# Attention weights left unnormalised: the reciprocal row sums multiply the outputs instead

## The chip, the cores and the metric

One core of one Trainium2 chip runs the whole kernel. The metric is the time of one execution on the device in microseconds (us), the median of several. Engines: TensorE (PE; its weight loads are PEld), VectorE (DVE), ScalarE (ACT), GpSimd (POOL) and SyncE (SP), each with an instruction queue of its own in program order, tied to the others by semaphores (`wait_ge`, `then_inc`).

## The reference

Three layers, one behind the other, on 2 x 768 tokens: attention with 8 heads of 64 per batch, then a gated mixture of 8 experts, then a gated pair of products. Cut to what matters here:

```python
def _attn_ref(q, k, v, n_sink, window):            # q, k, v: (2, 8, 768, 64)
    scores = scale * np.matmul(q, k.transpose(0, 1, 3, 2))
    keep = is_sink | in_window                     # first 4 keys, and the last 128
    scores = np.where(keep, scores, -1000000000.0)
    a = np.exp(scores - np.max(scores, axis=-1, keepdims=True))
    a = a / (np.sum(a, axis=-1, keepdims=True) + 1e-09)
    return np.matmul(a, v)
...
x = attn_out.transpose(0, 2, 1, 3).reshape(B * S, H * D)
x = _moe_ref(x, w_gate, w1, w2)                    # sum over experts of P * (relu(x @ w1) @ w2)
return _moe2_ref(x, w_a, w_b, w_out)               # (x @ w_a) * (x @ w_b) @ w_out
```

## The kernel before

**Pairs of heads.** Attention is done for 8 pairs of heads, `p` = 0 to 7 (`PAIRS`), pair `p` being heads 2i and 2i+1 (`a` = 0, 1) of batch b, with `i, b = divmod(p, 2)`. A pair has 6 tiles of 128 queries (`j`, `QT`); a tile sees 128 keys (j = 0) or 272 (the tile before, 16 sink keys, its own). Scores of tile j stand in PSUM banks 2*(j%2)+a, so banks 0 to 3; turned probabilities in banks 4 and 5 (`T_BANK`); outputs of the two halves of the sequence in banks 6 and 7 (`O_BANK`), head a in partitions 64a to 64a+63. `pr` is a ring of 4 (two pairs of two heads) with probabilities, `esum` holds their row sums, queries in the partitions.

**One pair's way.** ScalarE and VectorE split q and k into a rounded high part (`split_pair_hi`, L956 and L958) and a low part (`split_pair_lo`, L1258 and L1261). PE multiplies them (`scores`, L541), VectorE scales, masks and takes minima (`mask_scores`, L1272), ScalarE takes the exponentials in place with their row sums (`exps`, L967). VectorE adds 1e-9 and takes reciprocals, for two tiles at a time (`row_sums` L1284, `reciprocals` L1289). POOL multiplies the probabilities of tiles 0 to 2 (0 and 1 for the last pair) by them (`normalise`, L424), VectorE those of tiles 3 to 5 (L1298). PE turns the probabilities by transposes in four steps (`turn`, L567); ScalarE copies head 0's, VectorE head 1's into `pt` (`copy_turned`, L976 and L1307). PE multiplies them by the values (`weigh`, L588; sink keys L595), the two halves one after the other. ScalarE copies the outputs out of PSUM into their rounded high part (L982, L985) and issues the DMAs for the values of pair p+2 from its own queue (L988, L989). VectorE takes low parts and differences from the outputs in PSUM (`output_step`, L1317 to L1331), ScalarE rounds the differences (`token_parts_hi`, L997 to L1000), POOL takes their low parts (`token_parts_lo`, L449 to L456). These differences are operands of the expert products, which are done with seven block products instead of eight (P1 to P7), each of three matmuls per k (high by high, low by high, high by low; L623 to L625).

**The order by hand.** Every engine runs `pair(p)` for p from -2 or -1 on, and in it works on three pairs at once: outputs of p, turning of p+1, scores, masks and exponentials of p+2, the split of p+3. On PE: `weigh(p)`, then four times a turning step of p+1 followed by the scores of two tiles of p+2. On ScalarE: outputs of p; four times a turn copy and the exponentials of two tiles; the split of p+3; the rounding of differences of p. On VectorE: four times a turn copy, an output step, the masks of two tiles with sums and reciprocals between; the split of p+3; the last reciprocals; the six multiplications of tiles 3 to 5 of p+2. POOL: multiplications of p, the sink columns of k for p+2 (L414), low parts of p-2.

**What follows.** Behind the last pair PE does the first half of the router's logits (`logits_of(0)`, 20 matmuls, L648) and begins the experts (`group(0, 0)`): P1, P5, P2, P6, P3, P7 for the first half of the hidden columns, P1 of the second half, P4. P6 waits until ScalarE has copied P1's result out of PSUM (`keep`, L1071). The weights are split too: POOL makes sums of weight blocks (`weight_sums(n, sub)`, L436 to L441), ScalarE rounds them (`ws_hi`, L948), VectorE takes the low parts (`ws_lo`, L1336). The order of POOL at the end of attention is `weight_sums(0, 0)`, low parts of pair 6, `weight_sums(0, 1)`, low parts of pair 7.

Of the kernel before, what the change touches and what calls it, by code (L numbers as in the profile page):

```python
# [25 lines left out]
P = 128  # L26
# [7 lines left out]
def build(nc, qT, kT, v, sizes, w_gate, w1, w2, w_a, w_b, w_out, out):  # L34
# [43 lines left out]
    with ctx:  # L78
# [36 lines left out]
        with ExitStack() as att:  # L115
# [7 lines left out]
            mask = sa("mask", [P, MW], F32)  # L123
            wgs = sa("wgs", [P, KC, P], F32R)
# [22 lines left out]
        with ExitStack() as router:  # L147
# [10 lines left out]
            "sink_zero", "normed", "normed_dve", "turned", "turn_act", "turn_dve", "pv_done", "out_hi", "out_lo",  # L158
# [34 lines left out]
        def pool_tiles(p):  # L193
            return QT - 4 if p >= PAIRS - 1 else QT - 3

        def pool_before(p):
            return sum(2 * pool_tiles(x) for x in range(p))
# [6 lines left out]
        S_BANK, T_BANK, O_BANK = 0, 4, 6  # L204
        L_BANK = ((4, 5), (6, 7))
# [183 lines left out]
        def _(pool):  # L389
# [28 lines left out]
            def normalise(p, tiles):  # L418
                for j in tiles:
                    pool.wait_ge(s["recip"], 3 * p + 1 + j // 2)  # L420
                    for a in range(2):
                        r = 2 * (p % B) + a
                        t = pr[:, r, start_of[j]:start_of[j] + width[j]]
# [18 lines left out]

            def token_parts_lo(p):

                i, b = divmod(p, B)
                k = i % 2
                if i < 2:
                    pool.wait_ge(s["t_hi"], p + 1)
                    nc.gpsimd.tensor_tensor(xol[:, 4, k, b, :], x32[:, 5, k, b, :],  # L449
                                            xoh[:, 4, k, b, :].bitcast(F32), ALU.subtract).then_inc(s["t_lo"], 1)  # L450
                else:
                    pool.wait_ge(s["t_hi"], 4 + 2 * (p - 4) + 1)
                    nc.gpsimd.tensor_tensor(xol[:, 5:7, k, b, :], x32[:, 5:7, k, b, :],
                                            xoh[:, 5:7, k, b, :].bitcast(F32), ALU.subtract)
                    pool.wait_ge(s["t_hi"], 4 + 2 * (p - 4) + 2)
                    ins = nc.gpsimd.tensor_tensor(xol[:, 2, k, b, :], x32[:, 2, k, b, :],  # L456
                                                  xoh[:, 2, k, b, :].bitcast(F32), ALU.subtract)
                    if i == KC - 1:
                        ins.then_inc(s["x_ready"], 1)
# [27 lines left out]
            with pool.If(fits == 1):  # L487
                for p in range(B):
# [35 lines left out]
        def _(pe):  # L524
            pe.wait_ge(s["const_ready"], 15)

            def scores(p, tiles):
# [3 lines left out]
                for j in tiles:  # L531
                    bank = S_BANK + 2 * (j % 2)
                    pe.wait_ge(s["masked"], 2 * QT * p + 2 * j + 2)
                    at = max(j - 1, 0) * PITCH
# [11 lines left out]
            def turn(p, q):  # L546
                i = TURN_ORDER[q]
                for a in range(2):
# [13 lines left out]
                    for j, src, dst in parts:  # L562
                        if j < pool_tiles(p):
                            pe.wait_ge(s["normed"], pool_before(p) + 2 * j + a + 1)
                        else:
                            pe.wait_ge(s["normed_dve"], p + 1)
                        mm = nc.tensor.transpose(ps[:, bank, dst:dst + P], pr[:, r, src:src + P], ident[:])  # L567
                    mm.then_inc(s["turned"], 1)

            def weigh(p):  # L570
# [3 lines left out]
                for bank in range(2):  # L574
                    if p > 0:
                        pe.wait_ge(s["out_lo"], p)
# [61 lines left out]
            def logits_of(pi):  # L638

                if pi == 0:  # L640
                    pe.wait_ge(s["x_ready"], 1)
                    pe.wait_ge(s["gate_lo"], 1)
# [65 lines left out]
            with pe.If(fits == 1):  # L708
# [12 lines left out]
                for p in range(-1, PAIRS - 1):  # L721
                    if p >= 0:
                        weigh(p)
                    pair(p)
                weigh(PAIRS - 1)

# [196 lines left out]
        def _(act):  # L923
# [54 lines left out]
            def outputs(p):  # L978
                i, b = divmod(p, B)
                k = i % 2  # L980
                act.wait_ge(s["pv_done"], 2 * p + 1)
                nc.scalar.copy(xoh[:, i // 2, k, b, :], ps[:, O_BANK, 0:HT]).then_inc(s["out_hi"], 1)  # L982
                act.wait_ge(s["pv_done"], 2 * p + 2)
# [816 lines left out]
```

## Time and profile before

| | |
|---|---|
| time, median of 3 runs | 1452.02 us (1451.71 to 1453.65) |
| the profiled execution: its own time | 1450.18 us |
| the profiled execution: span from first to last instruction | 1448.4 us |
| busy over the span | PE 1398.6 us (97%), DVE 808.4 (56%), ACT 501.5 (35%), POOL 223.7 (15%) |
| mean granted TensorE clock | 0.997 |

A timeline row reads: start in us from the beginning of the span, duration in us (of all that are merged in it), engine, line of the kernel, operation, output<-inputs, forms, how many; in brackets the idle time of the engine just before and what ended it. L12 is line 12 of the kernel. A windows row reads: stretch, its length, then busy us and number of instructions for PE, PEld, DVE, ACT and POOL, the granted TensorE clock as a share of 2.4 GHz, the share of DMA time, and GB/s. Row groups by line read: busy us in all and mean ns of one, then idle time before them and who ended it. Matmuls overlap, so one's duration is longer than the distance to the next.

### The profile page before, as it was taken

To read this page: it belongs to the slowest core of one execution; us is meant where nothing else is said; L and a number is where in the kernel's file an instruction comes from. 1 tells how busy PE (TensorE), PEld (TensorE's weight loads), DVE (VectorE), ACT (ScalarE), POOL (GpSimd) and SP (SyncE) were. 2 spreads that over 40 slices of the span, in tenths; PEclk is the share of its full clock that TensorE was granted. 3 is DMA by queue.
4 is the path that set the end of the run, shared out by engine and by line. 5 is a ranking of instruction groups with operands and counts; after the bars stand their busy time and mean duration, and the time that the engine had idled before them with its cause. 6 is when DMAs were issued, how large, how long until landed. Compare 5 with 4: busy or idle time off the path is not lost.

```text
span 1448.4 us, 20715 instructions
## 1 busy us (share of the span) xinstructions
PE 1398.6 (97%) x7400; PEld 1246.1 (86%) x7400; DVE 808.4 (56%) x1585; ACT 501.5 (35%) x1085; POOL 223.7 (15%) x289
## 2 busy tenths in 40 slices
PE   4877999999999999999999999999999999999999
PEld 3655889988889998889998888998888989999998
DVE  6898765645444453544545444454544666656665
ACT  5785232423223242222323222242322443232331
POOL 3355110101101010110101011010111321101100
PEclk9999999999999999999999999999999999999999
DMA  4311100001010000101001010000100001001002
GB/s 141 100 45 56 44 30 29 30 29 59 15 44 29 29 29 29 58 21 37 29 29 32 26 58 29 29 29 29 58 15 29 15 30 44 30 30 44 30 1 88
DMA packets 49724, 56.45 MB, mean 39 GB/s; under 512 B 2432, under 2 KB 37376, under 8 KB 49664
## 3 DMA queue, kind: packets, MB, share of 16 engines
q1 hardware_dynamic: 44768, 53.26, 11.3%
q10 hardware_dynamic: 4896, 2.41, 0.6%
q8 instruction: 36, 0.59, 0.2%
q14 instruction: 24, 0.20, 0.0%
HBM read 52.51 MB, written 3.15 MB: 38 GB/s over the span
## 4 chain that ended last, share of the span: by engine, by line
PE 86%; DVE 7%; ACT 4%; issue 2%; DMA 0%; DVEq 0%; ACTq 0%
PE ps L623 28%; PE ps L625 28%; PE ps L624 28%; ACT pr L967 2%; DVE pr L1298 1%; DVE st L1675 1%; DVE pr L1272 1%; DVE wsl L1336 1%; PE ps L693 1%; DVE pt L1307 1%; ACT pt L976 1%; PE ps L567 0%; ACT st L1139 0%; ACT hh L1146 0%; DVE acc L1714 0%
## 5 line engine op out<-in xcount | busy, mean ns | idle before, releaser
L623 PE MATMUL ps<-xoh,wsh 128*128 128x384 f32 x1232 | 414.9, 337 | 3.0 <-DVE xol L1579 2.1
L625 PE MATMUL ps<-xol,wsh 128*128 128x384 f32 x1232 | 412.7, 335 | 0.0
L624 PE MATMUL ps<-xoh,wsl 128*128 128x384 f32 x1232 | 412.3, 335 | 0.0
L623 PE MATMUL ps<-w2h,hh 128*128 128x512 f32 x912 | 360.7, 396 | 0.8 <-DVE acc L1557 0.8
L625 PE MATMUL ps<-w2l,hh 128*128 128x512 f32 x912 | 359.8, 395 | 0.0
L624 PE MATMUL ps<-w2h,hl 128*128 128x512 f32 x912 | 359.6, 394 | 0.0
L1562 DVE SCALAR_TENSOR_TENSOR acc<-ps,g_now,acc 128x512 f32<-128x512 f32 x180 | 135.1, 751 | 201.7 <-PE ps L625 201.7
L623 PEld LDWEIGHTS ps<-xoh,wsh 128*128 128x128 f32 x1232 | 231.3, 188 | 10.5 <-DVE st L1675 3.9
L624 PEld LDWEIGHTS ps<-xoh,wsl 128*128 128x128 f32 x1232 | 231.3, 188 | 3.7
L625 PEld LDWEIGHTS ps<-xol,wsh 128*128 128x128 f32 x1232 | 231.2, 188 | 0.0
L625 PEld LDWEIGHTS ps<-w2l,hh 128*128 128x128 f32 x912 | 171.7, 188 | 39.8
L623 PEld LDWEIGHTS ps<-w2h,hh 128*128 128x128 f32 x912 | 171.9, 188 | 37.0 <-DVE acc L1557 1.2
L624 PEld LDWEIGHTS ps<-w2h,hl 128*128 128x128 f32 x912 | 171.8, 188 | 35.7
L436 POOL TENSOR_TENSOR sst<-raw 128x256 f32<-128x256 f32 x44 | 32.5, 738 | 1037.6 <-DVE wsl L1336 1037.6
L1071 ACT COPY st<-ps 128x384 f32<-128x384 f32 x96 | 46.0, 480 | 373.7 <-PE ps L625 373.7
L1535 DVE TENSOR_TENSOR st<-ps,st 128x384 f32<-128x384 f32 x96 | 53.4, 557 | 122.2 <-PE ps L625 122.2
L1535 DVE TENSOR_TENSOR ab<-ps,ab 128x384 f32<-128x384 f32 x96 | 53.5, 558 | 85.0 <-PE ps L625 84.9
L1543 DVE SCALAR_TENSOR_TENSOR hl<-ps,hh 128x384 fp32r<-128x384 f32 x64 | 35.7, 557 | 77.2 <-ACT hh L1084 76.7
L1336 DVE TENSOR_TENSOR wsl<-raw,wsh 128x512 fp32r<-128x512 f32 x88 | 63.8, 739 | 17.4 <-ACT wsh L948 17.4
L948 ACT CAST wsh<-raw 128x512 fp32r<-128x512 f32 x88 | 52.0, 621 | 55.2 <-POOL raw L438 55.2
L1084 ACT ACTIVATE hh<-ps 128x384 fp32r<-128x384 f32 x64 | 31.5, 491 | 106.1 <-PE ps L625 106.1
L1071 ACT COPY ab<-ps 128x384 f32<-128x384 f32 x96 | 46.1, 480 | 55.6 <-PE ps L625 55.6
(142 smaller groups left out, 1337.8 us busy)
## 6 DMA issues: line engine op xcount, KB each, us to landing
raw<-in_w_dram SPq DMA_DIRECT2D x32, 512.0 KB, 3.4
raw<-in_w_dram SPq DMA_DIRECT2D x16, 1024.0 KB, 5.1
rk<-in_k_dram SPq DMA_DIRECT2D x8, 384.0 KB, 4.0
rq<-in_q_dram SPq DMA_DIRECT2D x8, 384.0 KB, 4.9
raw<-in_w_a_dram SPq DMA_DIRECT2D x6, 512.0 KB, 3.6
raw<-in_w_b_dram SPq DMA_DIRECT2D x6, 512.0 KB, 3.6
raw<-in_w_out_dram SPq DMA_DIRECT2D x6, 512.0 KB, 3.5
out_dram<-acc SPq DMA_DIRECT2D x12, 256.0 KB, 2.0
```

The source lines that it names most:

```text
L436: nc.gpsimd.tensor_tensor(s1, a21, a22, ALU.add).then_inc(s["s_sum"], 1)
L623: nc.tensor.matmul(o, ah, bh, start=first, stop=False, skip_group_check=True)
L624: nc.tensor.matmul(o, al, bh, start=False, stop=False, skip_group_check=True)
L625: return nc.tensor.matmul(o, ah, bl, start=False, stop=last, skip_group_check=True)
L948: nc.scalar.copy(ws_piece(wsh, sub, j), ws_raw(sub, j)).then_inc(s["w_hi"], 1)
L967: nc.scalar.activation(t, t, ACT.Exp, bias=nmin[:, r, j:j + 1], scale=-1.0, accum_out=esum[:, r, j:j + 1]).then_inc(s["exped"], 1)
L1071: nc.scalar.copy((st, ab)[sub][:, slot, :], ps[:, bank_of(sub, name), 0:HT]).then_inc(s["kept"], 1)
L1084: nc.scalar.activation(hh[:, 2 * sub + 1, 0, :], ps[:, bank_of(sub, "P4"), 0:HT], ACT.Relu)\
L1336: nc.vector.tensor_tensor(ws_piece(wsl, sub, j), ws_raw(sub, j), ws_piece(wsh, sub, j).bitcast(F32), ALU.subtract)\
L1535: nc.vector.tensor_tensor(t, ps[:, bank_of(sub, name), 0:HT], t, ALU.add).then_inc(s["c_add"], 1)
L1543: nc.vector.scalar_tensor_tensor(out=hl[:, 2 * sub + m, half, :], in0=src, scalar=0.0, in1=hh[:, 2 * sub + m, half, :].bitcast(F32), op0=A ...
L1562: ins = nc.vector.scalar_tensor_tensor(out=acc[:, tile, :], in0=ps[:, Y_BANK + k % 2, :], scalar=g_now[:, tile:tile + 1], in1=acc[:, tile, ...
```

## The change

Nothing divides the probabilities any more: PE turns the exponentials as they are (`turn` waits for `exped`). Sums and reciprocals are done once for a pair, for all six tiles, `esum` then holding the reciprocals. A new step on PE, `widen(p)`, ahead of `weigh(p)`, has 12 matmuls whose weight is a column of `esum` broadcast to 64 columns and whose moved operand is the identity: the result has in the 64 rows of a head the reciprocal of each query's sum along the columns, in banks 2 and 3, which the scores of odd tiles use too (they wait for `wide_in`). VectorE begins `pair(p)` with `scale_outputs(p)`: it copies the 128x768 reciprocals into a new buffer `wide`, then multiplies the two halves of the outputs by it, from PSUM into `x32`. ScalarE rounds these from `x32` (one copy before its first turn copy, for p from 4 on another behind it), and issues the value DMAs behind the first turn copy. The differences of outputs and their low parts go from VectorE to POOL for p up to 5 (`output_sums`, `outputs_lo`), and stay on VectorE for the last two pairs (`output_sum`), where VectorE also takes the low parts of pair 6's differences; POOL takes the low parts of the outputs of pairs 6 and 7 behind `weight_sums(0, 0)` and ahead of `weight_sums(0, 1)`. POOL copies the sink columns three pairs ahead instead of two. The general path for other sizes is not run with these inputs.

```diff
@@ POOL
-            def normalise(p, tiles):
-                for j in tiles:
-                    pool.wait_ge(s["recip"], 3 * p + 1 + j // 2)
-                    for a in range(2):
...
-                        nc.gpsimd.tensor_scalar(t, t, esum[:, r, j:j + 1], None, ALU.mult)\
-                            .then_inc(s["normed"], 1)
+            def outputs_lo(p):
+                i, b = divmod(p, B)
+                k = i % 2
+                pool.wait_ge(s["out_hi"], p + 1)
+                pool.wait_ge(s["t_sum"], t_sums_before(p + 1))
+                ins = nc.gpsimd.tensor_tensor(xol[:, i // 2, k, b, :], x32[:, i // 2, k, b, :],
+                                              xoh[:, i // 2, k, b, :].bitcast(F32), ALU.subtract)
+                if i >= 2:
+                    ins = nc.gpsimd.tensor_tensor(xol[:, 3, k, b, :], x32[:, 3, k, b, :],
+                                                  xoh[:, 3, k, b, :].bitcast(F32), ALU.subtract)
+                ins.then_inc(s["out_lo"], 1)
+
+            def output_sums(p):
...
+                pool.wait_ge(s["scaled"], 2 * p + 2)
+                if i < 2:
+                    nc.gpsimd.tensor_tensor(t12, b12, early, ALU.subtract).then_inc(s["t_sum"], 1)
+                else:
+                    nc.gpsimd.tensor_tensor(t12, b22, t12, ALU.subtract).then_inc(s["t_sum"], 1)
+                    pool.wait_ge(s["t_sum"], t_sums_before(p) + 1)
+                    nc.gpsimd.tensor_tensor(t4, early, t12, ALU.subtract).then_inc(s["t_sum"], 1)
+                    nc.gpsimd.tensor_tensor(b12, b22, b12, ALU.subtract).then_inc(s["t_sum"], 1)
...
-                for p in range(PAIRS):
-                    own = range(pool_tiles(p))
-                    normalise(p, own[:2])
-                    if p + 2 < PAIRS:
-                        sink_columns(p + 2)
-                    normalise(p, own[2:])
-                    if p >= 2:
-                        token_parts_lo(p - 2)
+                for p in range(PAIRS - 2):
+                    if p + 3 < PAIRS:
+                        sink_columns(p + 3)
+                    output_sums(p)
+                    outputs_lo(p)
+                    token_parts_lo(p)
                 pool.wait_ge(s["qk_lo"], 2 * PAIRS)
                 weight_sums(0, 0)
-                token_parts_lo(PAIRS - 2)
+                outputs_lo(PAIRS - 2)
+                outputs_lo(PAIRS - 1)

             weight_sums(0, 1)
             token_parts_lo(PAIRS - 1)
@@ PE
-                        if j < pool_tiles(p):
-                            pe.wait_ge(s["normed"], pool_before(p) + 2 * j + a + 1)
-                        else:
-                            pe.wait_ge(s["normed_dve"], p + 1)
+                        pe.wait_ge(s["exped"], 2 * QT * p + 2 * j + a + 1)
...
+            def widen(p):
+                pe.wait_ge(s["recip"], p + 1)
+                pe.wait_ge(s["masked"], 4 + 2 * QT * min(p + 2, PAIRS))
+                for j in range(QT):
+                    at = j % 3 * P
+                    for a in range(2):
+                        r = 2 * (p % B) + a
+                        rows = slice(D * a, D * a + D)
+                        mm = nc.tensor.matmul(ps[rows, WIDE_BANK + j // 3, at:at + P],
+                                              esum[:, r, j:j + 1].to_broadcast([P, D]), ident[:],
+                                              start=True, stop=True, skip_group_check=True)
+                mm.then_inc(s["recip_wide"], 1)
@@ ScalarE
+                    if p >= 0 and q == 0:
+                        outputs_hi(p, True)
+                        next_values(p)
@@ VectorE
-            def normalise(p):
-                dve.wait_ge(s["recip"], 3 * p + 3)
-                for j in range(pool_tiles(p), QT):
-                    for a in range(2):
...
-                        ins = nc.vector.tensor_scalar(t, t, esum[:, r, j:j + 1], None, ALU.mult)
-                ins.then_inc(s["normed_dve"], 1)
+            def scale_outputs(p):
+                i, b = divmod(p, B)
+                k = i % 2
+                dve.wait_ge(s["recip_wide"], p + 1)
+                nc.vector.tensor_copy(wide[:], ps[:, WIDE_BANK:WIDE_BANK + 2, 0:HT]).then_inc(s["wide_in"], 1)
+                dve.wait_ge(s["wide_in"], p + 1)
+                for half, place in enumerate((i // 2, 2 + i // 2)):
+                    dve.wait_ge(s["pv_done"], 2 * p + half + 1)
+                    nc.vector.tensor_tensor(x32[:, place, k, b, :], ps[:, O_BANK + half, 0:HT], wide[:, half, :],
+                                            ALU.mult).then_inc(s["scaled"], 1)
...
             def pair(p):
+                if p >= 0:
+                    scale_outputs(p)
                 for q in range(4):
                     if p >= 0 and p + 1 < PAIRS:
                         copy_turned(p + 1, q)
-                    if p >= 0:
-                        output_step(p, q)
+                    if p >= PAIRS - 2:
+                        output_sum(p, q)
...
                 if p + 2 < PAIRS:
-                    row_sums(p + 2, 2)
+                    row_sums(p + 2)
                 if 2 <= p + 3 < PAIRS:
                     split_pair_lo(p + 3)
                 if p + 2 < PAIRS:
-                    reciprocals(p + 2, 2)
-                    normalise(p + 2)
+                    reciprocals(p + 2)
+                if p == PAIRS - 2:
+                    token_parts_lo(p)
```

## Rows read from the trace of the kernel before

**Rows 1.** The page: its first line and the chain that ended last, by engine.
```profile
span 1448.4 us, 20715 instructions
...
PE 86%; DVE 7%; ACT 4%; issue 2%; DMA 0%; DVEq 0%; ACTq 0%
```

**Rows 2.** Windows of all engines, then of PE alone: busy us, clock, DMA.
```profile
0.00:133.00 133.00, 93.18 (x780) 68.28 (x780) 110.71 (x376) 88.81 (x267) 58.14 (x88) 0.97 0.29 89
...
59.00:60.00 1.00, 1.00 (x7) 0.50 0.00 0
...
104.00:105.00 1.00, 0.00 (x0) 1.00 0.00 0
...
107.00:108.00 1.00, 1.00 (x13) 0.50 0.00 0
```

**Rows 3.** Timeline of ScalarE: start, duration, what it ran, idle time before it.
```profile
41.88 0.40 ACT L967 ACTIVATE pr<-pr,nmin 128x128 f32<-128x128 f32 x1 [0.82 <-DVE nmin L1272]
...
70.22 0.40 ACT L967 ACTIVATE pr<-pr,nmin 128x128 f32<-128x128 f32 x1 [1.90 <-DVE nmin L1272]
...
79.88 0.38 ACTq L988 DMA_DIRECT2D vs<-in_v_dram  x1
...
80.95 0.59 ACT L976 COPY pt<-ps 128x512 f32<-128x512 f32 x1 [0.59 <-PE ps L567]
...
83.99 0.40 ACT L967 ACTIVATE pr<-pr,nmin 128x128 f32<-128x128 f32 x1 [2.46 <-DVE nmin L1272]
...
113.24 0.40 ACT L967 ACTIVATE pr<-pr,nmin 128x128 f32<-128x128 f32 x1 [0.87 <-DVE nmin L1272]
...
144.11 0.84 ACT L1071 COPY st<-ps 128x384 f32<-128x384 f32 x2
```

**Rows 4.** Timeline of VectorE.
```profile
24.11 2.53 DVE L1298 TENSOR_SCALAR pr<-pr,esum 128x272 f32<-128x272 f32 x6
...
78.34 1.02 DVE L1258 TENSOR_TENSOR w2l<-rq,w2h 128x768 fp32r<-128x768 f32 x1 [0.71 <-ACT w2h L956]
...
80.44 2.25 DVE L1298 TENSOR_SCALAR pr<-pr,esum 128x272 f32<-128x272 f32 x6
...
82.60 0.68 DVE L1307 COPY pt<-ps 128x512 f32<-128x512 f32 x1
...
83.20 0.54 DVE L1317 TENSOR_TENSOR xol<-ps,xoh 128x384 fp32r<-128x384 f32 x1
...
121.23 6.04 DVE L1298 TENSOR_SCALAR pr<-pr,esum 128x272 f32<-128x272 f32 x8
```

**Rows 5.** Groups by line and form, 0 to 150 us.
```profile
L1307 DVE COPY pt<-ps 128x512 f32<-128x512 f32 x24 | 16.4, 683 | 2.7 <-PE ps L567 2.7
...
L456 POOL TENSOR_TENSOR xol<-x,xoh 128x384 fp32r<-128x384 f32 x4 | 5.0, 1255 | 0.0
...
L1307 DVE COPY pt<-ps 128x384 f32<-128x384 f32 x8 | 4.4, 545 | 2.2 <-PE ps L567 1.9
```

**Rows 6.** Timeline of PE.
```profile
36.94 0.39 PE L595 MATMUL ps<-pt,vz 128*64 128x128 f32 x4
37.16 1.47 PE L588 MATMUL ps<-pt,vs 128*64 128x128 f32 x16
...
58.05 1.82 PE L567 MATMUL ps<-ident,pr 128*128 128x128 f32 x8 [0.82 <-ACT pt L976]
...
93.53 1.09 PE L567 MATMUL ps<-ident,pr 128*128 128x128 f32 x8
...
138.06 0.45 PE L648 MATMUL ps<-xoh,wgs 128*128 128x384 f32 x1 [0.66 <-POOL xol L456]
...
149.20 0.44 PE L623 MATMUL ps<-xoh,wsh 128*128 128x384 f32 x1
```

**Rows 7.** Timeline of POOL.
```profile
121.86 1.96 POOL L453 TENSOR_TENSOR xol<-x,xoh 128x768 fp32r<-128x768 f32 x1 [1.89 <-ACT xoh L999]
...
138.96 0.74 POOL L436 TENSOR_TENSOR sst<-raw 128x256 f32<-128x256 f32 x1 [0.96 <-DVE wsl L1336]
```

More of the change, by code:

```diff
@@ L123, in build @@
             mask = sa("mask", [P, MW], F32)
+            wide = sa("wide", [P, 2, HT], F32)
             wgs = sa("wgs", [P, KC, P], F32R)
@@ L191, in build, with t_sums_before, t_parts_before @@
         TURN_ORDER = (0, 1, 3, 2)
[L193 to L197, printed above, removed]
+        def t_sums_before(p):
+            return min(p, 2 * B) + 3 * max(p - 2 * B, 0)
+        def t_parts_before(p):
+            return min(p, 2 * B) + 2 * max(p - 2 * B, 0)
         def chosen(eng):
@@ L204, in build @@
         S_BANK, T_BANK, O_BANK = 0, 4, 6
+        WIDE_BANK = 2
         L_BANK = ((4, 5), (6, 7))
@@ L441, in weight_sums @@
                 nc.gpsimd.tensor_tensor(s4, a12, s2, ALU.subtract).then_inc(s["s_sum"], 1)
+            def outputs_lo(p):
[12 more added lines that the diff above has]
+                k = i % 2
+                early, b12, b22, t12, t4 = (x32[:, o, k, b, :] for o in (i // 2, 2, 3, 5, 6))
+                pool.wait_ge(s["scaled"], 2 * p + 2)
[6 more added lines that the diff above has]
+                    nc.gpsimd.tensor_tensor(b12, b22, b12, ALU.subtract).then_inc(s["t_sum"], 1)
             def token_parts_lo(p):
@@ L533, in scores @@
                     pe.wait_ge(s["masked"], 2 * QT * p + 2 * j + 2)
+                    if j == 1 and p >= 2:
+                        pe.wait_ge(s["wide_in"], p - 1)
                     at = max(j - 1, 0) * PITCH
@@ L722, in _ @@
                     if p >= 0:
+                        widen(p)
                         weigh(p)
                     pair(p)
+                widen(PAIRS - 1)
                 weigh(PAIRS - 1)
+                pe.wait_ge(s["wide_in"], PAIRS)
             def unit_product(name, n, sub, pi):
@@ L976, in copy_turned, with outputs_hi, next_values @@
                 nc.scalar.copy(pt[:, 0, i, 0:w], ps[:, T_BANK, 0:w]).then_inc(s["turn_act"], 1)
-            def outputs(p):
+            def outputs_hi(p, late):
                 i, b = divmod(p, B)
                 k = i % 2
-                act.wait_ge(s["pv_done"], 2 * p + 1)
-                nc.scalar.copy(xoh[:, i // 2, k, b, :], ps[:, O_BANK, 0:HT]).then_inc(s["out_hi"], 1)
-                act.wait_ge(s["pv_done"], 2 * p + 2)
-                late = x32[:, 2, k, b, :] if i < 2 else xoh[:, 3, k, b, :]
-                nc.scalar.copy(late, ps[:, O_BANK + 1, 0:HT]).then_inc(s["out_hi"], 1)
+                if not late:
+                    act.wait_ge(s["scaled"], 2 * p + 1)
+                    ins = nc.scalar.copy(xoh[:, i // 2, k, b, :], x32[:, i // 2, k, b, :])
+                    if i < 2:
+                        ins.then_inc(s["out_hi"], 1)
+                elif i >= 2:
+                    act.wait_ge(s["scaled"], 2 * p + 2)
+                    nc.scalar.copy(xoh[:, 3, k, b, :], x32[:, 3, k, b, :]).then_inc(s["out_hi"], 1)
+            def next_values(p):
+                i, b = divmod(p, B)
                 if i + 1 < KC:
+                    act.wait_ge(s["pv_done"], 2 * p + 2)
                     cols = slice((i + 1) * P, (i + 2) * P)
@@ L1003, in pair @@
                 if p >= 0:
-                    outputs(p)
+                    outputs_hi(p, False)
                 for q in range(4):
@@ new lines, in output_sum @@
+            def output_sum(p, x):
+                i, b = divmod(p, B)
+                k = i % 2
+                early, b12, b22, t12, t4 = (x32[:, o, k, b, :] for o in (1, 2, 3, 5, 6))
+                if x == 0:
+                    dve.wait_ge(s["scaled"], 2 * p + 2)
+                    dve.wait_ge(s["t_lo"], p - 3)
+                    nc.vector.tensor_tensor(t12, b22, t12, ALU.subtract).then_inc(s["t_sum"], 1)
+                elif x == 1:
+                    dve.wait_ge(s["t_sum"], t_sums_before(p) + 1)
+                    nc.vector.tensor_tensor(t4, early, t12, ALU.subtract).then_inc(s["t_sum"], 1)
+                elif x == 2:
+                    nc.vector.tensor_tensor(b12, b22, b12, ALU.subtract).then_inc(s["t_sum"], 1)
```

73 lines of the change are left out of this document (27 added, 46 removed).

## The prediction, made before the change was run

> **What bounds the kernel now.** I read the page first: the chain of work that ended last is TensorE for 86% of a span of 1448.4 us, VectorE for 7%, ScalarE for 4%, and names no POOL [rows 1]. Then the windows: from 0 to 133 us, where attention is, PE is busy 93.18 of 133 us, VectorE 110.71, ScalarE 88.81 [rows 2]. So the diff can only act on when the stream of expert products begins; behind it everything moves by the same amount. Then the timelines of the three engines, to find the loop that sets a round (one head pair). I mark a round by the first exponential on ScalarE: 41.88, two rounds on 70.22, then 83.99 and, two rounds on, 113.24 us [rows 3]. A plain round is 13.77 us (70.22 to 83.99). It alternates: exponentials and turn copies on ScalarE until the q split of a later pair lets VectorE start its low part 8.12 us after the mark (78.34 against 70.22); the two low parts and the reciprocals take it to 80.40 [rows 3, 4]; six multiplications of probabilities on VectorE take 2.25 us (from 80.44), and the turn copy (0.60 from start to next start), one output subtraction (0.47) and the first masked scores (0.3) lead to the next mark [rows 4, 5]. POOL's multiplications and PE lie beside this. PE's first 8 transposes begin 9.54 us after a mark (93.53) and take about 1.03, while VectorE asks for them 12.38 after it (82.60): a slack of 1.8 us [rows 4, 6].
>
> **The steady round after.** Removed from this loop: the 2.25 us of multiplications and the 0.47 us output subtraction. Added on VectorE behind the reciprocals (10.2 us after the mark): a copy of 128x768 from PSUM. Copies of 128x512 and 128x384 take 683 and 545 ns [rows 5]; 138 ns for 128 elements makes about 0.95 us; bounds 0.68 (as for 512) and 1.09 (two of 384). It must land before the product reads it, then a product of 0.54 us [rows 4] gives the first half at 11.75. The second product costs 0.47, the turn copy 0.60, the first mask 0.3: VectorE would reach the mark at 13.1. ScalarE now waits for the first product instead of for PE: its copy 0.45 us (11.8 to 12.25), then the turn copy, and behind it the two value DMAs, moved from before the turn copy to after it. Those two issues hold ScalarE 1.05 us from the start of the instruction they are issued under (79.88 to 80.95) [rows 3]. This gives 13.3: ScalarE decides by 0.2 us. From the fifth pair on there is a second rounding copy there, 0.45 us: 13.75. If the issue is hidden a round is 13.1.
>
> PE gains 12 spreading matmuls a round, 64 columns wide, 128 moved. The trace has no such instruction with a broadcast weight; the nearest are the sink products of 128x128, 4 records (2 matmuls, one for each head) in 0.22 us from 36.94 to 37.16 [rows 6]. Twelve are six such pairs, 1.3 us. The first transposes then end near 11.7 us after the mark instead of 10.6, and VectorE asks for them at 12.2 (behind both products): 0.5 us of slack is left. If the two halves did not run together it is about 3.0 us, by 24 records at 0.13 us, the spacing of the 8 transposes of 128 [rows 6]. Nothing below 1.3 is likely; I take 1.3. The small sum and reciprocal instructions go from six to two, and lie under ScalarE's exponentials: nothing. The POOL work removed (46 multiplications) isn't in the chain [rows 1]: nothing. The POOL work added (one to three differences, low parts) lies after the products; its consumer, ScalarE's rounding of differences, comes 9 us later: nothing, except where it meets VectorE at the end.
>
> **The sum, stage by stage.** Start: the multiplications for pair 0 hold VectorE 2.53 us from 24.11 [rows 4]; without them the masks of pair 1 start 2.5 us earlier. Then the first spreading matmuls stand ahead of the first weighing and here PE has no slack, so 0.6 comes back. First mark 40.0, that is -1.9. Three plain rounds: before 42.11 (the first two 28.34, 0.8 over two plain ones: they hold a stretch where the granted clock was 0.50, the 1.2 GHz level [rows 2]), after 39.9: -2.2. Two late rounds: before 83.99 to 113.24, 29.25; after 27.5: -1.75. Mark at 107.4.
>
> The last pairs: before, the eight multiplications of the last pair took 6.04 us (against 2.25 for six), because POOL's subtractions from 121.86 on and VectorE's instructions with SBUF operands stood in each other's way, up to 127.27 [rows 4, 7]. After, the exponentials end at 114.4, ScalarE's roundings take 1.2 and the first weight piece 0.6; VectorE's weight piece then waits for POOL's 128x768 subtraction, about 117.5, and ends 118.2. Broad copy 0.95, products 1.0, turn copy 0.6: 120.7. Three more turn rounds of about 1.1, spreading 1.3 and weighing 3.3: 128.6. PE starts the first logits at 128.7 instead of 138.06 [rows 6]: -9.4.
>
> Not all of that stays. After the last weighing the order is: VectorE copy, two products, three differences, done near 132.6. POOL takes the low parts of the last outputs (two; 128x384 takes 1255 ns on average where VectorE meets it, I take 2.2 for both), and only then the sums of weights for the second half, four at 0.75 us [rows 5, 7]. Before, these sums stood ahead of the last token parts and began at 138.96, 0.9 us after the logits [rows 7]. With two waits of 0.6 us behind VectorE they now end near 139.1. ScalarE is in order: it rounds the last weight piece (0.8), and only then keeps P1 (0.45), which the fourth product P6 waits for. That is 140.35. PE reaches P6 after 20 logit matmuls (3.5 us) and three products (3.1 us): 135.3. It waits 5.05 us. Before, the keep began at 144.11 [rows 3] and P6 was reached at 138.06 + 6.6 = 144.7: no wait. So -9.4 becomes -4.4; the 0.3 us that PE then waited before the product at 149.20 [rows 6] is gone too: -4.7.
>
> **A pause of 5 us.** At 104 to 105 us PE did nothing, and at 107 to 108 its granted clock was 0.50, the 1.2 GHz level; at 59 to 60 it was low behind a wait of under 1 us [rows 2]. A longer pause makes a fall likelier. By the second such case, where 8 transposes took 1.82 us instead of 1.09 and two rounds 0.8 longer [rows 3, 6], a fall costs at least 0.8 us; I take twice that, 1.7, since PE alone would be the bound here. I take this in: -4.7 + 1.7 = -3.0 us.
>
> The Trainium skill (TensorE: Matmul & The Clock Gate, section "What's actually happening") says that TensorE's clock falls to 1.2 GHz when it has been idle long enough and comes back after sustained work. By it the fall is certain and the result -3.0; without the rule the sum would be -4.7. The trace is partly with it: the pause at 104 was followed by the low level, but the fall at 58 had no such pause ahead of it.
>
> The sum is made against the profiled execution (span 1448.4 us, its own time 1450.18 us). The median of the runs is 1452.02, so I forecast 1449.0 there, 1447.2 for a profiled execution like this one.
>
> **Rivals.** (a) The last stall is short: POOL and VectorE hardly meet, the clock stays, the issue of DMAs is hidden. Then 1.2 (POOL without its waits) and 1.7 (clock) come back, and five rounds at 13.1 instead of 13.3 give 1.0: -6.9 us, 1445.1. For it: VectorE's first product could start before POOL's work. Against: the weight sums stand behind the last outputs in POOL's order whatever the speeds. (b) The freed time is taken by the new order altogether: the opening stall is longer by 2 to 3 us, since each difference on VectorE and POOL waits for the other as in the 6.04 us row. Then -1 to 0 us, 1451.5: no measurable change. For it: that row. Against: it was three POOL instructions in a row. (c) Slower: the spreading matmuls aren't paired and become the bound. At 3.0 us the 1.7 more exceed the 0.5 of slack by 1.2, and the mark comes at 12.2 + 1.2 + 0.9 = 14.3 (turn copy and mask behind it), five of them +5.0, the start and the last weighing +1.7 each, of which the POOL chain carries all: -3.0 + 8.4 = +5.4 us, 1457.4. It decides from 1.8 us on (slack used up), and is slower than before from about 2.1. For it: a broadcast weight is unknown here. Against: pairs of head halves do overlap in the weighing rows. (d) That the probabilities' multiplications were hidden anyway is excluded by the chain: VectorE's six of them lie on it in each round.
>
> **Numbers.** My forecast 0.5 (own range 1447.0 to 1451.0); (a) 0.2; (b) 0.2; (c) 0.1. A measurement tells about 0.2%, 2.9 us. The forecast lies at that border; half of it and all of (a), and a little of the early gains, count as faster: 0.52; same: 0.35, from the rest of the forecast and (b); slower: 0.13, (c) and a longer stall than in (b). The range reaches from (a) to somewhat over no change: 1444.8 to 1453.2.
>
> **What would show it.** Rounds of 13.3 us between marks for plain pairs (14 or more: (c), 13.1: issue hidden); six pairs of spreading matmuls in 1.3 us; PE's first logit matmul near 128.7; a wait of PE of about 5 us at the fourth product, released by ScalarE's copy of P1, behind POOL's weight sums; a granted clock of 0.5 behind it; from then on the same span. The prediction is wrong if that wait is under 2 or over 8 us, if VectorE's copy of 768 takes over 1.3 us, or if a round is set by PE.

## The result, and the profile after

The changed kernel takes 1443.64 us, median of 4 runs (1443.19 to 1445.95), against 1451.87 us for the kernel before in 4 runs (1450.96 to 1453.65): a ratio of 0.995, 95% interval 0.9938 to 0.9962, or 8.2 us less. The forecast was 1449.0 us and its range ended at 1444.8, so the gain is larger than the range allowed. The profiled execution of the changed kernel took 1445.95 us, the longest of its four, and its span is 4.3 us shorter than in [rows 1]. One execution, of 2309.79 us at a mean granted clock of 0.562 (experiment 8, the others there 0.995 to 0.998), is left out of all medians and intervals.

The page: first line and the chain that ended last.
```profile
span 1444.1 us, 21020 instructions
...
PE 88%; DVE 5%; ACT 5%; issue 2%; POOL 0%; DMA 0%; DVEq 0%; POOLq 0%
```
Windows, of all engines and then of PE alone, for [rows 2].
```profile
0.00:133.00 133.00, 103.81 (x1042) 83.92 (x1043) 100.58 (x309) 91.29 (x272) 44.10 (x66) 1.00 0.30 93
...
137.00:142.00 5.00, 5.00 (x16) 0.50 0.33 108
```
In the first 133 us VectorE is busy for 10 us less, and PE for 10.6 us more, since the spreading matmuls, the first logits and the first expert products lie inside the stretch. The low clocks of [rows 2] at 59 and 107 us are gone: from 0 to 130 us the mean granted clock is 1.00 in all seven profiles of kernels with the change, and 0.97, 0.97 and 0.99 in the three without it (before, experiments 4 and 8). The 0.8 us that the low clock had added to the first two rounds before are part of the gain. A new stretch at half clock, the 1.2 GHz level, stands at 137 to 142.

Timeline of ScalarE, for [rows 3]: the marks, and the instructions ahead of one.
```profile
40.06 0.40 ACT L1004 ACTIVATE pr<-pr,nmin 128x128 f32<-128x128 f32 x1 [0.78 <-DVE nmin L1321]
...
64.35 0.51 ACT L1020 CAST xoh<-x 128x384 fp32r<-128x384 f32 x1 [2.30 <-DVE x L1353]
64.44 0.38 ACTq L1032 DMA_DIRECT2D vs<-in_v_dram  x1
64.77 0.58 ACT L1013 COPY pt<-ps 128x512 f32<-128x512 f32 x1
64.85 0.56 ACTq L1033 DMA_DIRECT2D vz<-in_v_dram  x1
65.62 0.40 ACT L1004 ACTIVATE pr<-pr,nmin 128x128 f32<-128x128 f32 x1 [0.27 <-DVE nmin L1321]
...
78.39 0.40 ACT L1004 ACTIVATE pr<-pr,nmin 128x128 f32<-128x128 f32 x1 [0.27 <-DVE nmin L1321]
...
103.79 0.56 ACTq L1033 DMA_DIRECT2D vz<-in_v_dram  x1
103.80 0.51 ACT L1025 CAST xoh<-x 128x384 fp32r<-128x384 f32 x1
104.40 0.40 ACT L1004 ACTIVATE pr<-pr,nmin 128x128 f32<-128x128 f32 x1
```
The marks are at 40.06, 52.84, 65.62, 78.39, 91.40 and 104.40. A plain round is now 12.78 us, 13.77 before. In it the DMA issues that were to hold ScalarE run in the shadow of its rounding and its turn copy, from 64.44 to 65.41; ScalarE then idles 0.27 us and is released by VectorE's mask. The two late rounds take 13.0. There the second rounding stands behind the turn copy, and the second issue ends at 104.35, 0.05 us ahead of the mark: ScalarE doesn't idle, and the mark comes 0.55 us after the start of VectorE's mask (103.85) instead of 0.32.

Timeline of VectorE in the same round, for [rows 4].
```profile
60.87 0.96 DVE L1307 TENSOR_TENSOR wsl<-rq,wsh 128x768 fp32r<-128x768 f32 x1 [0.92 <-ACT wsh L993]
61.74 1.03 DVE L1310 TENSOR_TENSOR wsl<-rk,wsh 128x848 fp32r<-128x848 f32 x1
62.70 0.22 DVE L1334 RECIPROCAL esum<-esum 128x12 f32<-128x12 f32 x1
62.83 0.89 DVE L1349 COPY wide<-ps 128x768 f32<-128x768 f32 x1
63.76 1.02 DVE L1353 TENSOR_TENSOR x<-ps,wide 128x384 f32<-128x384 f32 x2
64.70 0.68 DVE L1342 COPY pt<-ps 128x512 f32<-128x512 f32 x1
65.30 0.28 DVE L1321 CUSTOM_DVE_ANT_0 pr<-ps,mask 128x128 f32<-128x128 f32 x1
```
Only the first carries a wait in brackets, for ScalarE's rounding of q; from there to the mask at 65.30 VectorE works without a wait. So a plain round has two parts: ScalarE's, 8.0 us from the mark at 52.84 to the end of that rounding, without idle time and about as long as before (8.12), and VectorE's, 4.75 us from there to the next mark. In the rest of this text "VectorE decides" is meant of this second part.

Timeline of PE, for [rows 6]: the spreading matmuls, the first logits, the first wait among the expert products, and the logits turned, the last instruction that I use to measure what attention and opening cost together.
```profile
58.67 1.53 PE L598 MATMUL ps<-ident,esum 128*64 128x128 f32 x24
60.00 1.28 PE L621 MATMUL ps<-pt,vs 128*64 128x256 f32 x12
...
127.10 0.41 PE L682 MATMUL ps<-xoh,wgs 128*128 128x384 f32 x1 [1.15 <-DVE wide L1349]
...
133.62 0.34 PE L658 MATMUL ps<-xol,wsh 128*128 128x384 f32 x1
136.74 0.69 PE L656 MATMUL ps<-xoh,wsh 128*128 128x384 f32 x1 [2.78 <-ACT st L1120]
137.23 0.52 PE L657 MATMUL ps<-xoh,wsl 128*128 128x384 f32 x1
...
154.22 0.94 PE L690 MATMUL ps<-ident,lt 40*128 40x40 f32 x12 [0.52 <-DVE lt L1419]
```
The 24 records of twelve spreading matmuls take 1.33 us to the next group. The first logits come 10.96 us earlier than in [rows 6]. P6, the fourth product, waits 2.78 us, and behind the wait matmuls stand 0.32 us apart instead of 0.17.

What the wait was for is read from the chain between 128.9 and 136.7 us: start, duration, what.
```profile
128.93 0.48 DVE x L1369
...
130.51 1.01 POOL xol L447
131.52 1.16 POOL sst L431
...
134.25 1.20 POOL sst L436
...
135.48 0.83 ACT wsh L985
136.31 0.39 ACT st L1120
```
This is the chain that the prediction described: VectorE's last difference, POOL's low parts, POOL's sums of weights, ScalarE's rounding of the last weight piece, and only then its copy of P1.

Where the time went, by stages (forecast, and measured, against the profiled execution of before):

| place | before | after | forecast shift | measured shift |
|---|---|---|---|---|
| first mark | 41.88 | 40.06 | -1.9 | -1.8 |
| mark of the last pair | 113.24 | 104.40 | -5.85 | -8.8 |
| first logit matmul | 138.06 | 127.10 | -9.4 | -11.0 |
| P6 begins | 144.76 | 136.74 | -4.4 | -8.0 |
| logits turned | 159.71 | 154.22 | -3.0, with the clock's fall | -5.5, with it |

The last 1.2 us between -5.5 and the span's -4.3 lie far behind the change, where this execution has a stretch at a lower granted clock (mean 0.91 from 1165 to 1185 us). The low clock behind P6's wait costs this execution 2.8 us, nearly all of it in 18 matmuls at 0.32 us instead of 0.17. Without it the shift would be -8.3 us.

### The profile page after: what moved, and what is told of

Its sections match the earlier page's. It is cut to its first block, busy times and chain, and to the rows that moved or that the text cites. A ratio compares the mean times of both kernels' runs of the same rounds, so it can differ in the third digit from the quotient of the medians.

```text
span 1444.1 us, 21020 instructions
## 1 busy us (share of the span) xinstructions
PE 1404.1 (97%) x7592; PEld 1258.3 (87%) x7592; DVE 789.1 (55%) x1507; ACT 499.1 (35%) x1081; POOL 206.0 (14%) x263
## 4 chain that ended last, share of the span: by engine, by line
PE 88%; DVE 5%; ACT 5%; issue 2%; POOL 0%; DMA 0%; DVEq 0%; POOLq 0%
PE ps L656 29%; PE ps L658 28%; PE ps L657 28%; ACT pr L1004 2%; DVE st L1722 1%; ACT pt L1013 1%; PE ps L727 1%; DVE wide L1349 0%; PE ps L586 0%; ACT st L1188 0%; DVE pr L1321 0%; ACT hh L1195 0%; DVE wsl L1385 0%; DVE acc L1761 0%; DVE x L1353 0%
```

## The experiments

The theory from these rows: three terms were off. Rounds are set by VectorE at 12.78 us, not by ScalarE at 13.3, so the stream begins 3 us earlier (experiments 5 and 6). P6's wait is set by POOL's order (2 and 3). The fall of the clock that the forecast took in happens in a part of the executions only (1, and the others beside it). Rivals: ScalarE does decide (then 6 shortens a round and 5 does nothing); the gain has little to do with the division (4); it comes from POOL and VectorE meeting less (8); PE's new work is near its limit (7). The first four ran beside a kernel before of 1451.33 us, the others beside 1451.25 us; the changed kernel itself was not measured again beside 5 to 8.

**1. The changed kernel again, five executions.** No edit.

> The changed kernel once more, unchanged. Theory A: the gain is the sum of the stages seen in its trace, 11.0 us by the first logit matmul, less a pause of 2.8 us ahead of the fourth product, 8.0 to 8.3 us in a run in which the clock stays at 2.4 GHz behind the pause. In the one trace so far it fell to 1.2 GHz and 18 matmuls went at 0.32 us instead of 0.173, 2.6 us. Then the times have two levels, about 1443.5 and 1446. Rival B: the fall is a constant part of the change, and the lower times come from elsewhere: one level, and every profile has the slow stretch.

1442.42 us (1440.78 to 1443.75), ratio 0.9936 (0.9923 to 0.995). The same pause at P6 (2.81 us), and in the profiled execution (1443.75 us) the same fall: 0.83 is the mean clock from 130 to 150 us. The five have two levels, 2.7 us apart, though lower than expected: 1443.75 and 1443.52 us with a mean granted clock of 0.998, 1440.78 and 1441.02 with 1.000, and 1442.42 between them with 0.999. A fall like the profiled one, 5.8 us at half clock, lowers the mean by 0.002. So one and the same kernel runs with the fall and without it. With 1.000 there was no full one; that the low clock of 1443.52 stands at P6 too isn't shown. The four executions of the first measurement have 0.996 (the profiled one, with its two stretches), 0.999, 0.997 and 0.998.

**2. The sums of weights ahead of the last outputs on POOL.**

```diff
@@ POOL
                 weight_sums(0, 0)
                 outputs_lo(PAIRS - 2)
+                weight_sums(0, 1)
                 outputs_lo(PAIRS - 1)
-            weight_sums(0, 1)
```

> POOL makes the sums of the second weight half before the low parts of the last pair's outputs instead of after them. Theory A: these sums, rounded by ScalarE ahead of its copy of P1, are what PE waits for at the fourth product. The pause of 2.8 us goes, and with it the fall of the clock: 1440.8 us, 2.8 under the changed kernel. Rival C: ScalarE's own queue (rounding the last pair's outputs and differences) holds the copy of P1: then the pause shrinks by at most 1 us, 1443. Rival D: VectorE's low parts of the weights become the next wait, at the first product of the second half: a pause of 1 to 2 us there, 1442.

1440.70 us (1439.35 to 1441.0), ratio 0.9926 (0.9913 to 0.994), 1.7 us under the changed kernel measured beside it and the fastest of those that divide. Timeline of PE in this kernel, from the first logits to the logits turned, all rows with a wait:
```profile
126.07 0.41 PE L683 MATMUL ps<-xoh,wgs 128*128 128x384 f32 x1 [1.15 <-DVE wide L1350]
...
138.10 0.44 PE L657 MATMUL ps<-xoh,wsh 128*128 128x384 f32 x1 [1.01 <-DVE st L1583]
...
148.62 0.94 PE L691 MATMUL ps<-ident,lt 40*128 40x40 f32 x12 [0.53 <-DVE lt L1420]
```
The wait for P1's copy is gone, and so is the low clock (mean 1.00 from 130 to 150). From the first logits to their turning it is 22.55 us, 27.12 in the changed kernel: 2.8 less wait, 2.7 less fall, 1.0 given back in a wait for VectorE's combinations that the first wait had covered. The order of two POOL calls is shown to be the cause of the pause. In the medians 1.7 us come of it and not 4.6: 2.8 less 1.0 is what is left where the changed kernel doesn't have the fall, and by the clocks in 1 at least two of its five executions have no full one.

**3. The same, and PE's wait for the wide copy behind the logits.**

```diff
@@ PE
                 weigh(PAIRS - 1)
-                pe.wait_ge(s["wide_in"], PAIRS)
...
             logits_of(0)
+            with pe.If(fits == 1):
+                pe.wait_ge(s["wide_in"], PAIRS)
             group(0, 0, opening=True)
```

> As the kernel with the weight sums first, and PE's wait for VectorE's broad copy of the last pair stands behind the first logit matmuls instead of ahead of them (they write other banks). Theory A: the first logit matmul starts 1.1 us earlier, and if nothing waits in the opening the whole 1.1 us stay: 1439.7 us. Rival C: ScalarE's copy of P1 is now the bound, and the 1.1 us come back as a wait at the fourth product: same as without this edit.

1440.86 us (1440.01 to 1440.9), ratio 0.9927 (0.9914 to 0.9941): nothing gained over 2. The logits begin at 125.30 with no wait, and the time is lost again at three places of PE's timeline:
```profile
132.55 0.44 PE L657 MATMUL ps<-xoh,wsh 128*128 128x384 f32 x1 [0.39 <-ACT st L1122]
136.20 0.44 PE L657 MATMUL ps<-xoh,wsh 128*128 128x384 f32 x1 [0.23 <-DVE wsl L1387]
138.57 0.44 PE L657 MATMUL ps<-xoh,wsh 128*128 128x384 f32 x1 [1.04 <-DVE st L1584]
```
So in this order the 1.15 us wait for the wide copy, which the prediction had overlooked, cost nothing by itself: behind it the other engines are late by as much. (The marks of this execution lie 0.45 us later than in 2, and so do the logits turned: 149.09 against 148.62.)

**4. The kernel before without any division.** The calls of `normalise` are left out of the kernel before, so the outputs are never divided by the row sums.

```diff
-                    normalise(p, own[:2])
...
-                    normalise(p, own[2:])
...
-                            pe.wait_ge(s["normed_dve"], p + 1)
+                        pe.wait_ge(s["exped"], 2 * QT * p + 2 * j + a + 1)
...
-                    normalise(p + 2)
```

> The kernel before, with the multiplications of the probabilities left out and nothing put in their place: the outputs are not divided by the row sums, which changes the results. It is the change's removal alone. Theory A: on VectorE a round loses 2.25 us, 13.77 to 11.5, or stops near 11.7 where ScalarE's own work sets it; the start gains 2.5, the last pair about 6. In all 2.5 + 5 x 2.2 + 5 = 18 us: 1434 us, so that what the change adds costs about 10 us. Rival: the multiplications were largely hidden or PE sets the round at once: less than 10 us faster than before.

1437.21 us (1434.68 to 1437.85), ratio 0.99 (0.9885 to 0.9915), 14.1 us less than before. Plain rounds are 12.07 us and the last one 13.69. This is the whole price that the division had on the path, to within 1 or 2 us: the four executions lie between 1434.68 (mean clock 1.000) and 1437.85 (0.998), and the profiled one has low clocks of its own (0.97 from 0 to 130 us). The change gets 8.2 to 8.9 of it and gives 5 to 6 back in the wide copy, the two products and the spreading; I had thought that it was 18 and 10.

**5. The value DMAs issued ahead of the first turn copy.**

```diff
@@ ScalarE
                     outputs_hi(p, False)
+                    next_values(p)
                 for q in range(4):
...
                         outputs_hi(p, True)
-                        next_values(p)
```

> The changed kernel with the two value DMAs issued where the kernel before issues them, ahead of ScalarE's first turn copy. The prediction's step: the issues hold ScalarE 1.05 us wherever they stand, so the round (ScalarE's chain decides) stays the same. Theory A: where the change puts them they run under the copies and cost nothing, VectorE decides the round (12.78 us) and ScalarE has 0.27 us to spare; ahead of the turn copy they push it and PE's second transposes back by about 0.5 us: round 13.0 and up to 1.2 us slower in all, 1444.8.

1444.37 us (1444.01 to 1447.51), ratio 0.996 (0.9945 to 0.9975). Timeline of ScalarE:
```profile
64.96 0.51 ACT L1020 CAST xoh<-x 128x384 fp32r<-128x384 f32 x1 [2.31 <-DVE x L1353]
64.96 0.38 ACTq L1032 DMA_DIRECT2D vs<-in_v_dram  x1
65.38 0.56 ACTq L1033 DMA_DIRECT2D vz<-in_v_dram  x1
66.03 0.59 ACT L1013 COPY pt<-ps 128x512 f32<-128x512 f32 x1 [0.56 <-issue]
66.52 0.40 ACT L1004 ACTIVATE pr<-pr,nmin 128x128 f32<-128x128 f32 x1
```
Now ScalarE does decide in plain rounds too: it idles 0.56 us in the issue, the exponential waits for nothing else, and marks are 13.07 to 13.18 us apart in plain rounds, 13.5 or 13.6 in late ones. From first to last mark it is 66.5 us against 64.3. What the forecast took for the changed order belongs to this one, and even here it is 13.1 and not 13.3. The time alone would not show it, since it lies among those of the changed kernel; the marks do.

**6. The first rounding of outputs behind the turn copy.**

```diff
@@ ScalarE
-                if p >= 0:
-                    outputs_hi(p, False)
                 for q in range(4):
...
                     if p >= 0 and q == 0:
+                        outputs_hi(p, False)
                         outputs_hi(p, True)
```

> The changed kernel with ScalarE's rounding copy of the first output half put behind its first turn copy instead of ahead of it. The prediction's step: ScalarE's chain (first product, rounding, turn copy, DMA issue) decides the round, so the turn copy starts 0.45 us earlier, but the sum of ScalarE's work ahead of the exponentials is unchanged. Theory A: VectorE decides (copy, two products, turn copy, mask), so a round stays at 12.78 us and the total at 1443.6, within 0.5. Rival: PE's second transposes, which wait for ScalarE's turn copy, decide something: 0.3 to 0.5 us a round faster, 1441.5.

1442.57 us (1441.93 to 1443.74), ratio 0.994 (0.9925 to 0.9955). In plain rounds ScalarE is done 0.3 us earlier, its idle time before the mark grows from 0.27 to 0.56, and the round stays at 12.78:
```profile
65.80 0.40 ACT L1004 ACTIVATE pr<-pr,nmin 128x128 f32<-128x128 f32 x1 [0.56 <-DVE nmin L1320]
...
78.57 0.40 ACT L1004 ACTIVATE pr<-pr,nmin 128x128 f32<-128x128 f32 x1 [0.56 <-DVE nmin L1320]
...
90.97 0.56 ACTq L1033 DMA_DIRECT2D vz<-in_v_dram  x1
91.57 0.40 ACT L1004 ACTIVATE pr<-pr,nmin 128x128 f32<-128x128 f32 x1 [0.37 <-DVE nmin L1320]
```
With 5 this settles who sets the plain round: VectorE, by about 0.3 us. The late rounds stay at 13.0, and the last two rows say why. The second rounding is over at 91.20 here, and VectorE's mask began at 91.02, which by the 0.33 us of plain rounds would allow a mark at 91.35. The mark comes at 91.57, 0.04 us after the end of the second issue, though the bracket names VectorE. So in late rounds the issues in ScalarE's queue do decide, by 0.2 us.

**7. The spreading matmuls done twice.**

```diff
@@ PE
-                for j in range(QT):
+                for j in tuple(range(QT)) * 2:
```

> The changed kernel with the 12 spreading matmuls of a pair done twice (same result). They take 1.33 us in the trace. PE's first transposes end 0.3 us before VectorE asks for them. Theory A: each round is longer by 1.33 - 0.3 = 1.0 us, six rounds with the first, and the last weighing by 1.3: about 7 us slower than the changed kernel, 1450.9. This is the size the third rival of the prediction (unpaired matmuls) would have had. Rival: PE is not near the bound, and less than 2 us are lost.

1449.90 us (1447.95 to 1451.58, ten runs), ratio 0.9991 (0.9982 to 1.0): 1.3 us under the kernel before, where the changed one is 8.2 to 8.9 under it. PE's timeline:
```profile
60.49 2.84 PE L598 MATMUL ps<-ident,esum 128*64 128x128 f32 x48
63.13 1.28 PE L621 MATMUL ps<-pt,vs 128*64 128x256 f32 x12
```
48 records take 2.64 us, so 24 cost 1.31. The plain round becomes 13.90, 1.12 longer: of the slack that PE had, 0.5 by the forecast, 0.2 was there. PE and VectorE are almost equally late in the changed kernel.

**8. The kernel before, with POOL's last subtractions held until VectorE's multiplications are done.**

```diff
@@ POOL (kernel before)
+                    if p == PAIRS - 1:
+                        pool.wait_ge(s["normed_dve"], PAIRS)
                     if p >= 2:
                         token_parts_lo(p - 2)
```

> The kernel before, with one wait added: POOL takes the low parts of pair 5 (and what follows) only when VectorE has multiplied the last pair's probabilities. Theory A: the 6.04 us of those eight multiplications are mostly waits for POOL; alone they take about 2.5, PE turns the last pair 3.5 us earlier, and POOL, 4 us later with its low parts and weight sums, gives part of it back at the first weight piece: 1 to 3 us faster than before, 1450. Rival: the multiplications are as slow without POOL: no gain, or 2 us slower because POOL's work is late.

1450.00 us (ten runs of 1447.29 to 1452.06), ratio 0.9991 (0.9982 to 1.0). VectorE's timeline, for the last of [rows 4]:
```profile
121.85 2.26 DVE L1300 TENSOR_SCALAR pr<-pr,esum 128x272 f32<-128x272 f32 x8
```
The eight multiplications take 2.26 us instead of 6.04, so POOL beside them was the cause of the 3.8 us. The first logits come at 136.07 instead of 138.06, with the last mark 0.6 later than in [rows 3]. The time falls by 1.3 us, which is just at the edge of the noise (0 to 2.6 by the interval). Perhaps that much of the change's gain was to be had without it.

**The clock behind the same pause.** Five profiled executions have PE's pause of 2.78 to 2.81 us at P6. Their granted clock and the time from P6 to the logits turned:

| kernel | mean clock, 130 to 150 us | from P6 to the logits turned |
|---|---|---|
| changed | 0.83 | 17.48 us |
| 1, changed again | 0.83 | 17.45 |
| 6, rounding behind | 0.91 | 16.27 |
| 5, DMAs ahead | 1.00 | 14.66 |
| 7, spreading twice | 1.00 | 14.66 |

The row of PE's windows of the changed kernel, and behind it that of 5.
```profile
130.00:150.00 20.00, 17.22 (x83) 0.83 0.08 27
```
```profile
130.00:150.00 20.00, 17.19 (x100) 1.00 0.14 46
```
PE is busy for the same 17.2 of 20 us and does 100 matmuls in it instead of 83. The fall costs 2.8 us where it is full, 1.6 where it is shorter (in 6, from about 137.9 to 141.2), and nothing where it doesn't come. These are four kernels, and in the two without a fall P6 also stands later (139.11 and 143.03 us, the others 136.05 to 136.74); that it isn't the kernel that decides is said by the mean clocks in 1, not by this table.

## Why the prediction was wrong, by its steps

The direction and the chain up to P6 were forecast; which engine sets a plain round, and the size, were not: -3.0 us forecast, -8.2 measured. The sum of the corrections is worked out at P6's beginning, since everything behind it moves with it.

- **Steady round: the step that failed.** "This gives 13.3: ScalarE decides by 0.2 us." VectorE decides, with 12.78. Two errors went into it. The two DMA issues were taken to hold ScalarE for 1.05 us from the start of the turn copy. They do take that long, but in plain rounds they begin under the rounding ahead of it (rounding from 64.35, issues from 64.44 to 65.41), so they are over 0.21 us before the mark and cost nothing; experiment 5 puts them ahead of the turn copy and pays 0.3 to 0.4 us a round. And VectorE's items were summed 0.3 us too long, to 13.1: the wide copy begins 9.99 us after the mark, not 10.2, and from its start at 62.83 to the mark it is 2.79 where 0.95 + 0.54 + 0.47 + 0.60 + 0.3 made 2.9. In late rounds ScalarE does decide, as forecast, but with 13.0 and not 13.75: the first product ends 0.3 us earlier than forecast, and the second rounding (0.45 in the sum) runs beside the issues and not behind them. Three plain rounds end 1.6 us earlier than forecast and two late ones 1.5, together 3.1 (64.34 us from first to last mark, 67.4 forecast), and so do the logits' inputs and POOL's chain: -3.0 us, the first mark having come 0.1 late. Rival (a) had a part of this in it, with 13.1 and 1.0 us.
- **The opening's wait: right in place, cause and order, wrong in size.** Forecast 5.05 us with P6 at 140.35; measured 2.78 with P6 at 136.74. P6 came 3.6 us earlier, 3.0 by the rounds and 0.6 because POOL's low parts took 2.0 (forecast 2.2), the sums 3.96 (3 and two waits, 4.2) and the rest of the chain a little less. PE was at P6 only 1.3 us earlier than forecast (133.96 against 135.3), because of the overlooked 1.15 us wait for the wide copy; so the wait shrank by 2.3. It is the position of P6, not the length of the wait, that enters the sum.
- **The clock: taken as certain, and it isn't.** 1.7 us were taken in. The fall came behind the pause as said and cost 2.8 us in the changed kernel (1.7 forecast), but two of five profiles with the same pause have none, and two of five executions of the changed kernel have a mean clock of 1.000. The term should have had a chance of its own. The Trainium skill (TensorE: Matmul & The Clock Gate, section "What's actually happening") says that the gate's own timing runs freely and isn't tied to the kernel. By that the same pause may or may not be followed by a fall, and the five profiles agree; its rule that idleness drops the clock was read in the prediction as if it were certain.
- **The sum.** For the logits turned in the profiled execution, which has the fall: -3.0 forecast, -3.0 for the rounds, -0.6 for the chain behind them, +1.1 for a fall of 2.8 and not 1.7, together -5.5 us; measured -5.5. Without a fall it would be -8.3. That the medians differ by nearly this, 8.2, is in part luck: by their clocks some of the four executions can have a fall, and the median before lies 1.7 us above the profiled execution from which the sum was made. How the 2.7 us between -5.5 and -8.2 are shared between the two isn't shown.
- **What held.** The start (-1.8 for -1.9). The spreading matmuls in pairs, 1.33 us for 1.3, so rival (c)'s premise is excluded; its threshold, slower from 2.1 us on, was too low with the rest of the sum: with 2.64 us in experiment 7 the kernel isn't slower than before. The wide copy, 0.91 us on average for 0.95. Nothing contradicts that POOL's multiplications and the small instructions cost nothing, but neither was tested by itself. That the division lay on the path: without any of it the time is 14.1 us less and a plain round 1.7 (experiment 4), which excludes (d).
- **The meeting of POOL and VectorE.** The forecast counted the 6.04 us as a loss that the change removes; experiment 8 shows that it was one, of which 2.0 us arrive at the first logits and about 1.3 in the time. It overlooked that the same meeting stands in the rounds. VectorE's timeline of before, in the last round:
```profile
108.14 3.80 DVE L1298 TENSOR_SCALAR pr<-pr,esum 128x272 f32<-128x272 f32 x6
```
Six multiplications take 3.80 us here, beside POOL's low part of 128x768 from 107.68 on, and 2.25 in plain rounds, also beside a POOL low part (79.60 to 81.17). At the pace of experiment 8, eight in 2.26, six would take 1.7, by estimate; so a part of the 2.25 in the prediction's loop is the meeting too. In the changed kernel they still meet, on VectorE's timeline here, but for less than (b) supposed:
```profile
113.35 1.48 DVE L1385 TENSOR_TENSOR wsl<-raw,wsh 128x512 fp32r<-128x512 f32 x1 [1.59 <-ACT wsh L985]
...
122.99 1.36 DVE L1379 TENSOR_TENSOR xol<-x,xoh 128x384 fp32r<-128x384 f32 x1
124.27 0.68 DVE L1385 TENSOR_TENSOR wsl<-raw,wsh 128x512 fp32r<-128x512 f32 x1
```
The weight piece takes 1.48 us beside POOL and 0.68 without it, and the subtraction of 128x384 takes 1.36 where others of that size take 0.56. The Trainium skill (SBUF — State Buffer, section "Who interferes with whom") names the port pair that VectorE and GpSimd share as the only place of contention. The 2.26 us of experiment 8 against 6.04 agree that the two hinder each other; that it is the only such place no run here shows.

Open is what decides whether the pause is followed by a fall, and how often it is: the mean clocks of nine executions are too few to count by. That the issues hold the late rounds is read from the rows of two kernels (the changed one and 6); a run with the issues taken out of late rounds alone was not made.

## What to carry to other kernels

When two engines finish a round within 0.3 us of each other by your sum, work out both cases as forecasts of their own, since an error in it is multiplied by the number of rounds; here the rounds were 3 of the 5.2 us that the forecast missed, about half in the plain ones. A DMA issue cost ScalarE's queue here only what no running instruction covered: look at what runs while it is issued and at what stands ahead of it, not at its own duration. The same two issues cost nothing in plain rounds, 0.2 us in late ones, with one more copy in the queue, and 0.3 to 0.4 ahead of the turn copy. When loop-end work moves between engines, write out the in-order queue of each engine at the join: the fastest version here differs from the change in the order of two calls on an engine that the chain hardly names.

## What the hardware showed that was not expected

The same pause of 2.8 us on PE was followed by the 1.2 GHz level in three of five profiles and not in the other two, at a cost from 0 to 2.8 us; the executions of one kernel show both. Eight 128x272 multiplications on VectorE took 6.04 us beside POOL's subtractions and 2.26 alone. Two DMA issues of 0.97 us together, in ScalarE's queue, delayed the next exponential by 0, 0.2 or 0.3 to 0.4 us, by their place in it. And a weight that is one column broadcast to 64 costs PE no more than an ordinary one of that size: 24 records of 128 moved columns in 1.31 to 1.33 us, 12 matmuls for two heads side by side.
